# SyncE waits for the queries and keys of the first four units before it issues the first values

## The reference

```python
# attention: a pooled path and a local path, summed
q_d, k_d, v_d = mean over groups of 4 tokens of q, k, v
out_up    = repeat(softmax(q_d @ k_d.T / 8) @ v_d, 4 tokens each)
mask      = |i - j| < 4
out_local = softmax(where(mask, q @ k.T / 8, -1e9)) @ v
x = out_up + out_local                     # seen as 2304 tokens x 512
# first feed-forward layer, 512 -> 2048 -> 512
x = elu(x @ w_in) @ w_out
# second feed-forward layer, 512 -> 1536 -> 512
x = (silu(x @ w_gate) * (x @ w_val)) @ w_out2
```

## Time and profile before

| what | value |
|---|---|
| median of three executions | 973.29 us |
| the profiled execution, its time | 971.3 us |
| its span in the trace | 969.5 us |
| PE busy | 959.9 us, 99% of the span |
| DVE, ACT, POOL busy | 604.1, 385.6, 163.4 us |
| TensorE clock granted | full, the whole span by the page |
| DMA moved | 67.88 MB, mean 70 GB/s |

### The profile page before, as it was taken

How to read it: one execution, slowest core, us unless ns; L and a number is a source line. 1 busy time by engine, 2 the same in 40 slices (tenths; PEclk the granted TensorE clock), 3 DMA queues, 4 the chain that set the end, 5 groups by cost and what they waited for, 6 DMA issues and landing times.

```text
span 969.5 us, 20170 instructions
## 1 busy us (share of the span) xinstructions
PE 959.9 (99%) x7916; PEld 908.1 (94%) x7917; DVE 604.1 (62%) x1364; ACT 385.6 (40%) x1027; POOL 163.4 (17%) x210
## 2 busy tenths in 40 slices
PE   8999999999999999999999999999999999999998
PEld 5889999999999999999999999999999999999998
DVE  7887656566555565555358884534759846667552
ACT  5776554344344443444335632232324422222221
POOL 7304510014000000000006920000008910000000
PEclk9999999999999999999999999999999999999999
DMA  9645531125110211110132301112023132120202
GB/s 250 186 127 109 99 58 47 27 73 106 27 39 26 75 51 31 60 37 8 56 108 87 99 23 44 45 44 67 1 87 123 58 103 88 44 87 23 88 11 77
DMA packets 55661, 67.88 MB, mean 70 GB/s; under 512 B 6760, under 2 KB 37832, under 8 KB 55568
## 3 DMA queue, kind: packets, MB, share of 16 engines
q1 hardware_dynamic: 48272, 62.76, 21.0%
q0 software_dynamic: 6816, 3.55, 2.7%
q10 hardware_dynamic: 480, 0.30, 0.1%
HBM read 52.42 MB, written 14.16 MB: 69 GB/s over the span
## 4 chain that ended last, share of the span: by engine, by line
PE 94%; ACT 3%; DVE 2%; DMA 1%; issue 1%; ACTq 0%; DVEq 0%
PE bank L572 29%; PE bank L573 28%; PE bank L574 28%; PE bank L536 2%; PE bank L500 2%; PE bank L521 2%; PE bank L558 1%; PE bank L512 1%; ACT weights L1104 1%; DMA q_sb<-qT 1%; DVE weights L793 1%; ACT prob L1060 1%; PE bank L546 0%; PE bank L487 0%; DVE g_sb L818 0%
## 5 line engine op out<-in xcount | busy, mean ns | idle before, releaser
L574 PE MATMUL bank<-x_hl,gv_hl 128*128 128x256 f32 x768 | 217.3, 283 | 0.0
L573 PE MATMUL bank<-x_hl,gv_hl 128*128 128x256 f32 x768 | 217.3, 283 | 0.0
L572 PE MATMUL bank<-x_hl,gv_hl 128*128 128x256 f32 x768 | 217.2, 283 | 0.0
L572 PE MATMUL bank<-x_hl,weights 128*128 128x384 f32 (+1 forms) x448 | 147.2, 329 | 2.0 <-DVE weights L793 1.8
L572 PEld LDWEIGHTS bank<-x_hl,gv_hl 128*128 128x128 f32 x768 | 147.3, 192 | 0.9
L573 PEld LDWEIGHTS bank<-x_hl,gv_hl 128*128 128x128 f32 x768 | 147.3, 192 | 0.9
L572 PE MATMUL bank<-g_hl,weights 128*128 128x384 f32 (+1 forms) x448 | 147.8, 330 | 0.3 <-DVE g_hl L827 0.2
L1315 POOL TENSOR_TENSOR gv_hl<-gv_raw,gv_hl 128x256 fp32r<-128x256 f32 x84 | 72.5, 898 | 447.9 <-ACT gv_hl L1110 447.9
L574 PEld LDWEIGHTS bank<-x_hl,gv_hl 128*128 128x128 f32 x768 | 147.3, 192 | 0.0
L573 PE MATMUL bank<-x_hl,weights 128*128 128x384 f32 (+1 forms) x448 | 143.4, 320 | 0.0
L574 PE MATMUL bank<-g_hl,weights 128*128 128x384 f32 (+1 forms) x448 | 143.3, 320 | 0.0
(11 more groups left out here) (127 smaller groups left out, 1604.8 us busy)
## 6 DMA issues: line engine op xcount, KB each, us to landing
landing<-w SPq DMA_DIRECT2D x32, 256.0 KB, 4.8
x_raw<-yT_scratch SPq DMA_DIRECT2D x14, 512.0 KB, 4.5
v_win<-v_windows SPq DMA_DIRECT2D x46, 105.0 KB
q_sb<-qT SPq DMA_DIRECT2D x88, 48.0 KB, 2.3
partT_scratch<-out_sb SPq DMA_DIRECT2D x16, 256.0 KB, 2.2
out_sb<-partT_scratch SPq DMA_DIRECT2D x4, 1024.0 KB, 5.1
outT<-out_sb SPq DMA_DIRECT2D x16, 256.0 KB, 2.0
k_sb<-kT SPq DMA_DIRECT2D x14, 288.0 KB, 3.4
```

The costliest lines, as they stand in the source:

```text
L572: nc.tensor.matmul(out, w_hi, x_hi, start=first, stop=False)
L573: nc.tensor.matmul(out, w_hi, x_lo, start=False, stop=False)
L574: return nc.tensor.matmul(out, w_lo, x_hi, start=False, stop=last)
```

## The change

SP waits, after it has issued the queries and keys that are its own, for the landing of the queries and keys of units 0 to 3, those that ACT issued among them, and only then goes on with its list. Nothing else differs; all other lists and all data stay as they are. The four calls are four waits on four semaphores, each for 48 counts.

```diff
             for u in range(PROLOGUE):
                 load_k(sp, u)
             load_q(sp, 2)
+
+            for u in range(PROLOGUE):
+                wait_qk(sp, u)
             load_vraw(sp, ORDER_V[0])
             load_vwin(sp, 0)
             load_vraw(sp, 0)
```

## The result

The changed kernel takes 976.35 us in the median of 19 executions (970.59 to 978.5), the kernel before 971.46 us in as many beside it (969.82 to 974.42). The ratio on record is 1.0031, with a 95% interval of 1.002 to 1.0043: slower by 0.3%. The forecast of 975.5 is 0.9 us from the median, and its range holds it; the sum behind it does not hold, as the profile shows. The profiled execution took 976.25 us, its span is 974.4.

What follows compares the result with a forecast made beforehand. PE is busy 99% of the span, so only the start, a string of single waits before 28 us, could change the time. One term, +2.2 us for ACT's late copy, on 973.3 gave 975.5 us, range 971.5 to 977.8.

Steps and rivals of the forecast that it cites:

- the sum behind it: +2.2 us from ACT's late copy of unit 1 at 19.23, all else covered, added to a median of 973.3.
- The wait costs SP 5.6 us (4.0 to 6.0): SP's prologue: its first values start at 9.8 instead of 4.2, and the list queued behind moves by 5.6 us.
- My end of 9.8: SP's wait: unit 3's last query lands at 9.8 us, taken near the row of 10.2, not 8.2.
- The rule quoted: DMA queues: each engine takes turns between rings with work; a semaphore's count lands only behind that engine's earlier writes.
- Piece 0 lands 4.5 us behind its issue and the copy comes 2.2 late: ACT: weight piece 0, issued at 16.3, lands at 20.8; unit 1's copy starts at 21.4 instead of 19.23.
- The Trainium skill's estimate of 2.6 us: Piece 0's landing: about 2.0 us fixed plus bytes at 436 GB/s; the copy would start at 19.5, 0.3 late.
- my row: Piece 0's landing time: 4.5 us, from the piece issued at 31.2 behind three small DMAs.
- What is won does not add: Unit 1's queries on PE come 0 to 1.8 us sooner, but this only lengthens the stall behind piece 0.
- The clock, 0.05 and 1.5 us: Rival near 20 us: PE's longer standing halves the clock for 3 us, costing 1.5 more, 977.0; chance 0.05.
- All else covered: Values and later pieces arrive in time or are absorbed; SP's delay ends at its next own wait, 31.4; no added loss.
- piece 4, which I called in time: Pieces 4 to 9 land from 28.5 on; ACT rounds piece 4 at 29.1 at the earliest.
- 2.0 us below the median: The profiled execution of 971.3 lies 2.0 below the 973.29 median, so the forecast started from 973.3.

Runs made afterwards that it cites:

- the twelve profiles above: Profiles with POOL's take-up of unit 2: four without a wait on SP (9.26 to 10.09 us), eight with one (7.82 to 9.07).
- the fifth: Changed kernel with weight pieces 0 to 3 each issued earlier among the values on SP; 972.12 us, ratio 1.0009 to the kernel before.

## Why the prediction was right in its number and wrong in its reason

That 975.5 came so near 976.35 is luck. It held 1.8 us too much for the time before the change and 1.9 us too much for the late copy, and it left out the 4.6 us that the median lost to the clock.

- *The wait costs SP 5.6 us (4.0 to 6.0).* Measured 4.5 at the first values and 5.3 at piece 0. My end of 9.8 rested on the belief that the queries wait mostly behind themselves. Unit 3's last query took 4.7 us instead of 6.3, and the wait ended at 8.7. The rule quoted from the Trainium skill's "DMA: Bandwidth & Descriptors", section "Queues, rings and completion order", spoke for this, and unit 2's take-up in the twelve profiles above agrees with what it implies; which of its two mechanisms acts is not shown.
- *Piece 0 lands 4.5 us behind its issue and the copy comes 2.2 late.* This is the term of the sum that failed: 0.3 instead of 2.2. The place was right: the longest idle time of ACT there, 2.25 us, is put down to this DMA. The size was not. It took 3.0 us, with the DMA engines at a share of 0.69 from 16 to 18 us where the earlier trace rows have 0.98, and 16.0 + 3.0 + 0.5 gives 19.5. The Trainium skill's estimate of 2.6 us, quoted from the same page under "Anatomy of one DMA", was nearer than my row, though the page gives that fit for DMAs that GpSimd issues, and these are SP's.
- *What is won does not add.* Right for the copy, and I had said that the stall on PE would only be longer: about 2 us more. It was 1.4 more. PE is done with its transposes 1.1 us sooner and the copy is 0.3 later, so PE stood 1.72 us against 0.34 before. What I missed is that this longer stall has a price of its own.
- *The clock, 0.05 and 1.5 us.* This was the step that decided. I looked at the share of 1.00 behind an earlier wait of 1.31 us and took it for a licence. The fall came in two executions of three, lasted over 13 us instead of 3, and cost some 5. Filling the gap takes the cost away, and making the gap elsewhere brings it.
- *All else covered.* Right for the values: PE's L546 came at 16.04, sooner than before, and waited for none. The delay of SP's list met its next own wait as said, but at 35.4, not 31.4, since PE was at half clock. But piece 4, which I called in time, had 0.6 us of room by my own numbers; ACT stood for it in six of the experiments, and in the fifth that made the ELU late.
- *2.0 us below the median.* The 973.29 of three executions was high; 19 gave 971.46. The forecast of +2.2 met +4.9 between the medians, or +3.0 (1.9 to 4.2) by the ratio, made of something else. With the late copy right and the clock left out I would have said 971.8 from the median of 19, or 973.6 from the one I had.

## What to carry to other kernels

A wait that is put into a queue to help one load makes all behind it late; ask which of them stands ahead of something urgent in an in-order engine's list, and wait for as little as gives the gain. Where PE is kept busy by filler, do not count a new idle stretch of PE near it at its own length alone: here 1.72 us cost 5 behind it, in most executions, and 0.75 us cost nothing that shows. When a median rises by less than the spread of the executions, look at each execution's clock and time: a loss that comes in some of them only is not the steady cost that a sum of waits gives.

## What the runs showed of the hardware

- A gap on PE of 1.72 us, in a stretch of 2 us with 0.44 busy, was followed by about 13.6 us at half clock in the profile, and 13 of 19 executions have a mean clock of 0.995 or less; with one of 2.23 us all six have 0.993 or less. With 0.75 us none of eleven has 0.995 or less. The same stretch with 1.95 busy kept 1.00. The length of a gap is not all: the wait of 1.31 us before 8.79 was followed by 1.00.
- The kernel before is not free of it: of 81 executions run beside the experiments 4 have a mean clock of 0.995 or less, the worst 977.69 us, and 23 more have 0.996 or 0.998. Two of those took 977.25 and 976.95 us at 0.998, a loss that their clock doesn't explain and that stays open. At 1.0 the times scatter by 2.4 us, 969.8 to 972.2.
- A 256 KB load landed in 3.0 us with the DMA engines at a share of 0.69, and in 6.2 with 0.98. So of the 5.3 us by which piece 0 was issued later 3.2 were given back, and it landed 2.1 us later.
